# Sparse attention and two gated convolution layers: another order of a tile's transfers on the SyncE queue

## The chip, the core and the metric

The kernel runs on one core of one Trainium2 chip. The metric is the device time of one execution in microseconds. All work is issued by five engines that run side by side and meet only at semaphores: TensorE (PE), VectorE (DVE), ScalarE (ACT), GpSimd (POOL) and SyncE (SP), which here issues nearly all transfers between the chip's memory (HBM) and the on-chip memory.

## What is computed

`reference()` runs three layers one after the other. q, k and v have 2 batches, 8 heads, 768 rows and a head width of 64, in float32.

```
scores = scale * q @ k.T - slope[h] * dist              # keep: the first 8 keys and the last 96
a = exp(scores - max); a = a / (sum(a) + 1e-9); x = a @ v
x = (sigmoid(causal_conv5(x)) * (x @ w_val)) @ w_out    # layer 2, width 512
h = relu(x @ w_in)                                      # layer 3, width 1024
out = (h * sigmoid(conv3(h))) @ w_out2
```

The change touches only how the softmax's divisor, 1 / (sum(a) + 1e-9), travels to the result of attention, and when q, k and v are loaded.

## The kernel before

**Tiles.** Attention runs over TILES = 12 tiles of 128 query rows, tile t = 0 to 11, six for each batch. A tile has 8 heads (H) in 4 pairs (PAIRS). Its keys are 32 global ones, 96 of the previous tile and its own 128; tiles 0 and 6, the first of their batches, use their own 128 alone. q, k, v and the previous tile's rows of v stand in rings of RING = 4 slots, so tile t + 4 may be loaded when tile t has let go of its slot.

**The loop on each engine.** The order on every engine is written out by hand; no scheduler moves anything.

- PE, tile t: `qk(t + 1)` (scores of the next tile, L504), four `turn(t, j)` (transposes of the probabilities of tile t, L517), `pv(t)` (probabilities times v, L532). `pv(t)` takes the four pairs in turn and waits for each pair's copy of the turned probabilities, `probT`.
- DVE, tile t: `take_x(t - 1)` (L977, attention's result out of PSUM into `xT`), then the eight `score(t + 1, i)` (L954), and between them `inverse(t)` (L965 `total_eps`, L967 reciprocal), `turn_inverse(t)` (L973, a transpose of the inverses into `inv_rows`) and `copy_t1(t, 1)` (L961, the copy of pair 1 for which `pv(t)` waits). `copy_t1(t, 1)` stands behind `turn_inverse(t)`. Tiles 6 to 10 end with one or two steps of the first convolution (L982, `EARLY_STEPS`: 1, 2, 1, 2, 1), which read two operands from on-chip memory.
- ACT: eight exponentials of tile t + 1 (L701) and the copies of the other pairs (L708); from tile 5 on it copies pair 3 too.
- POOL, tile t: `key_window(t + 3)` (L389 and L390; waits for that tile's k), `split_w2` in tiles 0 to 3 or `split_x` in tiles 6 to 9 (L410, L412), then `scale_x(t - 1)` (L396, waits for the spread inverses `invT`; it multiplies them into `xT`, which is counted by `x_ready`).
- SP: the transfers, below.

**An inverse's way.** The inverses of a tile are 8 numbers for each of 128 query rows, one query row a partition. `xT` has the head's channels on the partitions, so they have to be turned and repeated. DVE transposes them into `inv_rows` (two slots, by t % 2). SP sends these rows to HBM, to `inv_turned` (L312, 16 KB; called the **send** below). When that has landed (semaphore `inv_sent`), SP reads them back twice, each time repeated over 64 partitions, into `invT` (L317, 2 x 128 KB; called the **spread**). DVE's `turn_inverse(t)` writes the slot that tile t - 2 sent from, and so waits until `inv_sent` of tile t - 2 has come.

**SP's queue.** It is in order: an instruction that waits holds up all behind it. For tile t it issues `load_q(t + 4)` (L293, waits for PE's `qk(t)`), `load_k(t + 4)` (L298, waits for the first half of `qk(t + 1)`), the send and the spread of tile t (`turn_inverse`), then `load_v(t + 4)` (L304, and for all but a batch's first tile L306 and L307; it waits for `pv(t)`). From tile 2 on the spread also waits for `scale_x(t - 2)`, the last reader of its slot.

**After attention** PE runs `val`, `hid` and `out` (products in three parts each, L561 to L563) to the end.

The functions that the change touches, with the lines of the profile:

Of the kernel before, what the change touches and what calls it, by code (L numbers as in the profile page):

```python
# [10 lines left out]
TILES = B * TPB  # L11
# [11 lines left out]
RING = 4  # L23
# [18 lines left out]
def program(nc, A_q, A_k, A_v, A_n, A_wval, A_w1t, A_win, A_w2, A_cw1, A_cw2, A_out):  # L42
# [7 lines left out]
    with ctx:  # L50
# [161 lines left out]
        def banded(eng):  # L212
            eng.wait_ge(n_in, 16)
            low_g, high_g, low_l, high_l = (eng.value_load(nw[0:1, i:i + 1]) for i in range(4))
            return (high_g == 0) & (high_l == 0) & (low_g >= 0) & (low_g <= GLOB) & (low_l >= 1) & (low_l <= PREV)
# [43 lines left out]
        def invT_of(t):  # L259
            return kW[:, 0, t % 2, :, :] if t >= LATE_INVERSES else invT[:, t % 2, :, :]  # L260

        def first_of_batch(t):
            return t % TPB == 0
# [16 lines left out]
        @block.sync  # L280
        def _(sp):
            sp.dma_start(win[:, 0, 0:F // 4], A_win[:, 0, 0:F // 4]).then_inc(start_in[0], 16)
            sp.dma_start(w1t[:, 0, P:C], A_w1t[:, 0, P:C]).then_inc(start_in[1], 16)
            for m in range(1, CT):
                sp.dma_start(w1t[:, m, :], A_w1t[:, m, :]).then_inc(w1_in[m], 16)
            sp.dma_start(wval, A_wval).then_inc(wv_in, 16)
            sp.dma_start(win[:, :, F // 2:F], A_win[:, :, F // 2:F]).then_inc(win_in, 16)


            def load_q(t):  # L290
                if t >= RING:
                    sp.wait_ge(qk_done, 2 * (t - RING) + 2)
                sp.dma_start(q_rows[:, t % RING, :, :], A_q[:, t, :, :]).then_inc(q_in[t % RING], 16)  # L293

            def load_k(t):
                if t >= RING:
                    sp.wait_ge(qk_done, 2 * (t - RING) + 3)
                sp.dma_start(kW[:, t % RING, 1, :, :], A_k[:, t, :, :]).then_inc(k_in[t % RING], 16)  # L298

            def load_v(t):  # L300
                if t >= RING:
                    sp.wait_ge(pv_done, t - RING + 1)
                slot = t % RING
                sp.dma_start(v_own[:, slot, :], A_v[:, t, :]).then_inc(v_in[slot], 16)  # L304
                if not first_of_batch(t):
                    sp.dma_start(v_win[GLOB:P, slot, :], A_v[GLOB:P, t - 1, :]).then_inc(v_in[slot], 16)  # L306
                    sp.dma_start(v_win[0:GLOB, slot, :], A_v[0:GLOB, t // TPB * TPB, :]).then_inc(v_in[slot], 16)  # L307

            def turn_inverse(t):
                slot = t % 2  # L310
                sp.wait_ge(inverse_done, t + 1)
                sp.dma_start(inv_turned[t].rearrange("h (b q) -> b h q", q=SQUARE), inv_rows[:, slot, :]).then_inc(inv_sent[slot], 16)  # L312
                sp.wait_ge(inv_sent[slot], 16 * (t // 2 + 1))
                if t >= 2:
                    sp.wait_ge(x_ready, t - 1)
                for e in range(2):
                    sp.dma_start(invT_of(t)[e * D:(e + 1) * D, :, :], inv_turned[t, e:H:2, :].partition_broadcast(D)).then_inc(invT_in[slot], 16)  # L317

            def load_w2(k):
                sp.dma_start(w2[:, k, :], A_w2[:, k, :]).then_inc(w2_in[k], 16)  # L320

            def general_load(m, first=False):
                tile = g_batch(m) * TPB
                pair = g_pair(m)
                if not first:
                    sp.wait_ge(g_pv, 2 * m)
                    sp.sem_inc(loading, 1)
                for e in range(2):
                    rows = slice(e * D, (e + 1) * D)
                    sp.dma_start(gq[:, e, :], A_q[rows, ds(tile + g_tile(m), 1), ds(pair, 1), :].rearrange("p t h s -> p (t h s)")).then_inc(g_in, 16)  # L330
                    sp.dma_start(gk[:, e, :, :], A_k[rows, ds(tile, TPB), ds(pair, 1), :].rearrange("p t h s -> p t (h s)")).then_inc(g_in, 16)
                sp.dma_start(gv[:, :, :], A_v[:, ds(tile, TPB), ds(2 * D * pair, 2 * D)]).then_inc(g_in, 16)

            with sp.If(banded(sp)):
                for t in range(RING):
                    load_q(t)
                    load_k(t)
                    load_v(t)
                for k in range(FT):
                    load_w2(k)  # L340
                for t in range(TILES):
                    if t + RING < TILES:
                        load_q(t + RING)
                        load_k(t + RING)
                    turn_inverse(t)
                    if t + RING < TILES:
                        load_v(t + RING)
            with sp.Else():
                sp.wait_ge(wvl_done, CT)
                general_load(0, first=True)  # L350
                for k in range(FT):
                    load_w2(k)
                with sp.Fori(1, G_STEPS) as m:
                    general_load(m)

            def store(c, ms):
                sp.wait_ge(o_free, CT * c + ms.stop)
                sp.dma_start(A_out[:, c, ms, :], ost(c)[:, ms, :]).then_inc(out_sent[c], 16)

            for c in range(CHUNKS - 1):  # L360
                store(c, slice(0, 2))
                store(c, slice(2, 4))
            store(CHUNKS - 1, slice(0, 2))
            store(CHUNKS - 1, slice(2, 3))
            store(CHUNKS - 1, slice(3, 4))
            for c in range(CHUNKS):
                sp.wait_ge(out_sent[c], 32 if c < CHUNKS - 1 else 48)
# [870 lines left out]
```

## Time and profile before

| | us |
|---|---|
| median of three runs | 277.49 |
| lowest, highest | 277.28, 278.51 |
| the profiled execution | 274.83 |
| its span, first to last instruction | 273.0 |
| PE busy | 261.7 (96%) |
| DVE busy | 185.8 (68%) |
| ACT busy | 155.3 (57%) |
| POOL busy | 47.7 (17%) |

All durations below come from the profiled execution, and times of day are microseconds from the start of its span. The busy shares are means over stages with different limits: attention ends at about 102 us, and the rest is PE's products. The rows on which the prediction rests are in a section of their own below.

### The profile page before, as it was taken

How to read it: one execution, taken by the hardware profiler on the slowest of the kernel's cores; microseconds unless marked ns; L12 is line 12 of the kernel's file. 1: busy time of each engine (PE TensorE's matmuls, PEld its weight loads, DVE VectorE, ACT ScalarE, POOL GpSimd, SP SyncE). 2: the span in 40 equal slices, each digit the busy share in tenths (PEclk: the TensorE clock that was granted, in tenths of full speed). 3: DMA queues.
4: the chain of work that ended last, by engine and by line, in shares of the span. 5: the costliest groups of instructions: out<-in, count | busy, mean ns of one | idle time of the engine just before them, and what ended most of it. 6: DMA issues, size and time to landing. Idle time of an engine off the chain costs nothing.

```text
span 273.0 us, 4415 instructions
## 1 busy us (share of the span) xinstructions
PE 261.7 (96%) x1526; PEld 205.4 (75%) x1526; DVE 185.8 (68%) x460; ACT 155.3 (57%) x353; POOL 47.7 (17%) x70
## 2 busy tenths in 40 slices
PE   8999999999977699999999999999999999999995
PEld 7444468888755588888888888888888888888883
DVE  0389399997966694698980696997508998992000
ACT  1051578889977686526451706765718748754110
POOL 1012095772254553400000000000000000000000
PEclk9999999999999999999999999999999999999999
DMA  6999716656554552100000000000000002104021
GB/s 196 365 379 316 289 42 197 194 162 182 160 158 133 169 145 83 45 0 0 2 0 0 0 2 0 0 0 1 2 0 0 0 2 87 67 0 155 1 90 64
DMA packets 20263, 25.16 MB, mean 92 GB/s; under 512 B 3728, under 2 KB 10384, under 8 KB 20112
## 3 DMA queue, kind: packets, MB, share of 16 engines
q1 hardware_dynamic: 19088, 23.86, 27.0%
q10 hardware_dynamic: 1152, 1.01, 1.1%
q8 instruction: 13, 0.21, 0.3%
q14 instruction: 10, 0.08, 0.1%
HBM read 21.52 MB, written 3.34 MB: 91 GB/s over the span
## 4 chain that ended last, share of the span: by engine, by line
PE 84%; DMA 8%; SPq 3%; DVE 2%; ACT 1%; issue 1%; ACTq 1%; DVEq 0%
PE ps L561 20%; PE ps L562 20%; PE ps L563 20%; PE ps L457 8%; PE ps L532 6%; PE ps L504 5%; PE ps L517 5%; DMA inv_turned<-inv_rows 4%; DMA win<-in_win 3%; SPq L317 1%; DVE prob L954 1%; SPq L304 0%; DVE probT L961 0%; SPq L298 0%; ACT prob L701 0%
## 5 line engine op out<-in xcount | busy, mean ns | idle before, releaser
L701 ACT ACTIVATE prob<-prob,low 128x256 f32<-128x256 f32 (+1 forms) x96 | 46.1, 483 | 10.5 <-DVE low L954 10.4
L982 DVE SCALAR_TENSOR_TENSOR g<-xT,cw,g 128x512 f32<-128x512 f32 x48 | 33.7, 767 | 1.6 <-ACT g L736 1.6
L810 ACT ACTIVATE h<-ps 128x512 f32<-128x512 f32 x24 | 14.0, 595 | 31.1 <-PE ps L563 31.1
L954 DVE CUSTOM_DVE_ANT_0 prob<-ps,bias 128x256 f32<-128x256 f32 x80 | 30.1, 409 | 1.7 <-PE ps L504 1.5
L561 PE MATMUL ps<-gh,Wh 128*128 128x512 f32 x64 | 24.9, 389 | 0.0
L562 PE MATMUL ps<-gl,Wh 128*128 128x512 f32 x64 | 24.9, 389 | 0.0
L563 PE MATMUL ps<-gh,Wl 128*128 128x512 f32 x64 | 24.9, 389 | 0.0
L561 PE MATMUL ps<-hghA,w2h 128*128 128x512 f32 x64 | 24.9, 389 | 0.0
L562 PE MATMUL ps<-hglA,w2h 128*128 128x512 f32 x64 | 24.9, 389 | 0.0
L563 PE MATMUL ps<-hghA,w2l 128*128 128x512 f32 x64 | 24.9, 389 | 0.0
L457 PE MATMUL ps<-win,w1t 128*128 128x512 f32 x56 | 24.7, 596 | 0.1
L1145 DVE SCALAR_TENSOR_TENSOR hgA<-h,cw,hgA 128x512 f32<-128x512 f32 x32 | 21.8, 745 | 3.6 <-ACT hgA L822 3.6
L517 PE MATMUL ps<-ident,prob 128*128 128x128 f32 x176 | 23.3, 278 | 0.6 <-ACT probT L708 0.5
L517 PEld LDWEIGHTS ps<-ident,prob 128*128 128x128 f32 x176 | 18.8, 140 | 5.9 <-issue 3.5
L504 PE MATMUL ps<-kW,q_rows 64*128 64x256 f32 (+1 forms) x192 | 22.3, 372 | 0.0
L532 PE MATMUL ps<-probT,v_win 128*64 128x128 f32 x160 | 16.3, 282 | 5.6 <-DVE probT L961 5.6
L457 PEld LDWEIGHTS ps<-win,w1t 128*128 128x128 f32 x56 | 10.5, 190 | 13.1 <-issue 12.0
L504 PEld LDWEIGHTS ps<-kW,q_rows 64*128 64x128 f32 x192 | 16.6, 186 | 4.6 <-issue 2.5
L708 ACT ACTIVATE probT<-ps 128x512 f32<-128x512 f32 (+1 forms) x31 | 17.2, 555 | 3.8 <-PE ps L517 3.7
L561 PE MATMUL ps<-xh,wvh 128*128 128x512 f32 x48 | 19.0, 396 | 0.0
L532 PE MATMUL ps<-probT,v_own 128*64 128x128 f32 x192 | 18.4, 276 | 0.6 <-DVE probT L961 0.4
L563 PE MATMUL ps<-xh,wvl 128*128 128x512 f32 x48 | 18.7, 390 | 0.0
(101 smaller groups left out, 530.6 us busy)
## 6 DMA issues: line engine op xcount, KB each, us to landing
q_rows<-in_q SPq DMA_DIRECT2D x12, 256.0 KB, 4.6
kW<-in_k SPq DMA_DIRECT2D x12, 256.0 KB, 4.4
v_own<-in_v SPq DMA_DIRECT2D x12, 256.0 KB, 3.7
invT<-inv_turned SPq DMA_DIRECT2D x20, 128.0 KB, 2.9
out<-xT SPq DMA_DIRECT2D x5, 512.0 KB, 2.8
w<-in_w SPq DMA_DIRECT2D x8, 256.0 KB, 10.0
v_win<-in_v SPq DMA_DIRECT2D x10, 192.0 KB, 3.4
prob<-in_wval SPq DMA_DIRECT2D x1, 1024.0 KB, 9.9
```

What stands on the lines that cost most here:

```text
L457: return pe.matmul(WB(i), w1t[:, m, k * P:(k + 1) * P], win[:, m, half * 512:(half + 1) * 512], start=(m == 0), stop=(m == CT - 1))
L504: last = pe.matmul(SC(f, i % 2)[:, i // 2, P if first_of_batch(t) else 0:KEYS], q_rows[rows, slot, pair, :], keys, start=True, stop=True)
L517: last = pe.transpose(PT(t, j)[:, (2 * i + c) * P:(2 * i + c + 1) * P], prob[:, t % 2, 2 * j + i, c * P:(c + 1) * P], ident[:, :])
L532: last = pe.matmul(PO[e * D:(e + 1) * D, j, :], v[:, slot, cols], probT[:, j // 2, j % 2 * 2 + e, c, :], start=(c == key_parts(t)[0]), sto ...
L561: pe.matmul(out, w_hi, x_hi, start=first, stop=False)
L562: pe.matmul(out, w_hi, x_lo, start=False, stop=False)
L563: return pe.matmul(out, w_lo, x_hi, start=False, stop=final)
L701: act.activation(part, part, ACT.Exp, scale=-1.0, bias=low[:, t % 2, i:i + 1], accum_out=total[:, t % 2, i:i + 1]).then_inc(exp_done, 1)
L708: act.activation(turned_to(t, j), turned(t, j), ACT.Copy).then_inc(t0_copied, 1)
L954: dve.tensor_tensor_reduce(prob[:, t % 2, i, cols], SC(f, e)[:, i % HH // 2, cols], table, -SCALE, 3.0e38, ALU.add, ALU.min, low[:, t % 2, ...
L982: dve.scalar_tensor_tensor(out=pieces(g[:, m, :], c), in0=x_cols(m, c, tap - PAD1), scalar=cw1[:, m, tap:tap + 1], in1=pieces(g[:, m, :], ...
L1145: dve.scalar_tensor_tensor(out=raw, in0=h_cols(m, c, tap - 1), scalar=cw2[:, m, tap:tap + 1], in1=raw, op0=ALU.mult, op1=ALU.add).then_inc ...
```

## The change

The transfers of a tile stand in another order on SP. Nothing is added or removed; the instructions on PE, DVE, ACT and POOL and their waits are as before.

```diff
-            def turn_inverse(t):
+            def send_inverse(t):
                 slot = t % 2
                 sp.wait_ge(inverse_done, t + 1)
                 sp.dma_start(inv_turned[t].rearrange("h (b q) -> b h q", q=SQUARE), inv_rows[:, slot, :]).then_inc(inv_sent[slot], 16)
+
+            def spread_inverse(t):
+                slot = t % 2
                 sp.wait_ge(inv_sent[slot], 16 * (t // 2 + 1))
                 if t >= 2:
                     sp.wait_ge(x_ready, t - 1)
...
                 for t in range(TILES):
+                    send_inverse(t)
+                    if t >= 1 and t - 1 + RING < TILES:
+                        load_v(t - 1 + RING)
                     if t + RING < TILES:
                         load_q(t + RING)
                         load_k(t + RING)
-                    turn_inverse(t)
-                    if t + RING < TILES:
-                        load_v(t + RING)
+                    spread_inverse(t)
```

The start of the loop on SP, tile 0 and tile 1, before:

```order
L293 DMA q_rows<-in_q 128x512 [waits qk_done]
L298 DMA kW<-in_k 128x512 [waits qk_done]
L312 DMA inv_turned<-inv_rows 4x32x32 [waits inverse_done]
L317 DMA invT<-inv_turned 64x4x128 [waits inv_sent0]
L317 DMA invT<-inv_turned 64x4x128
L304 DMA v_own<-in_v 128x512 [waits pv_done]
```

The same place after the change:

```order
L312 DMA inv_turned<-inv_rows 4x32x32 [waits inverse_done]
L293 DMA q_rows<-in_q 128x512 [waits qk_done]
L298 DMA kW<-in_k 128x512 [waits qk_done]
L320 DMA invT<-inv_turned 64x4x128 [waits inv_sent0]
L320 DMA invT<-inv_turned 64x4x128
L312 DMA inv_turned<-inv_rows 4x32x32 [waits inverse_done]
```

The send of tile 0 has moved ahead of the loads of q and k of tile 4, and the v of tile 4 now comes behind the send of tile 1.

From tile 1's spread to tile 2's, in the steady part of the loop on SP, before (the later tiles with loads have the same pattern; where the v is that of tile 6 it is L304 alone):

```order
L317 DMA invT<-inv_turned 64x4x128 [waits inv_sent1]
L317 DMA invT<-inv_turned 64x4x128
L304 DMA v_own<-in_v 128x512 [waits pv_done]
L306 DMA v_win<-in_v 96x512
L307 DMA v_win<-in_v 32x512
L293 DMA q_rows<-in_q 128x512 [waits qk_done]
L298 DMA kW<-in_k 128x512 [waits qk_done]
L312 DMA inv_turned<-inv_rows 4x32x32 [waits inverse_done]
L317 DMA invT<-inv_turned 64x4x128 [waits x_ready,inv_sent0]
L317 DMA invT<-inv_turned 64x4x128
```

The same place after the change:

```order
L320 DMA invT<-inv_turned 64x4x128 [waits inv_sent1]
L320 DMA invT<-inv_turned 64x4x128
L312 DMA inv_turned<-inv_rows 4x32x32 [waits inverse_done]
L304 DMA v_own<-in_v 128x512 [waits pv_done]
L306 DMA v_win<-in_v 96x512
L307 DMA v_win<-in_v 32x512
L293 DMA q_rows<-in_q 128x512 [waits qk_done]
L298 DMA kW<-in_k 128x512 [waits qk_done]
L320 DMA invT<-inv_turned 64x4x128 [waits x_ready,inv_sent0]
L320 DMA invT<-inv_turned 64x4x128
```

Before, nothing stood between a send and the spread that waits for its landing; now five loads do, and they wait for `inverse_done` of the tile in front of them.

## Rows read from the trace of the kernel before

**Rows 1.** The page, part 2: busy tenths of PE in 40 equal slices.

```profile
PE   8999999999977699999999999999999999999995
```

**Rows 2.** Stretches by engine: us, busy us (x instructions), PEclk, DMA share, GB/s.

```profile
72.00:96.00 24.00, 18.15 (x193) 14.54 (x192) 16.77 (x68) 18.74 (x63) 11.73 (x15) 1.00 0.56 168
...
112.00:270.00 158.00, 157.82 (x696) 130.32 (x695) 108.22 (x151) 79.36 (x110) 1.77 (x4) 1.00 0.05 20
```

**Rows 3.** Waits from 68 to 120 us: total us, times, longest.

```profile
DVE inv_rows L973 <- DMA inv_turned<-inv_rows: 6.9, 3, 2.3
...
PE ps L532 <- DVE probT L961: 5.6, 3, 2.1
```

**Rows 4.** Timeline of PE: start, us, instruction, idle time before it.

```profile
72.22 2.00 PE L504 MATMUL ps<-kW,q_rows 64*128 64x256 f32 x16
...
78.64 0.44 PE L532 MATMUL ps<-probT,v_win 128*64 128x128 f32 x4 [1.45 <-DVE probT L961]
...
96.32 2.00 PE L504 MATMUL ps<-kW,q_rows 64*128 64x256 f32 x16
...
102.30 0.50 PE L561 MATMUL ps<-xh,wvh 128*128 128x512 f32 x1
```

**Rows 5.** The chain of waits, 73 to 90 us: start, us, what.

```profile
73.49 3.88 DMA inv_turned<-inv_rows
...
77.38 0.61 SPq L317
...
78.03 0.62 SPq L317
...
78.70 0.60 SPq L304
...
79.34 0.43 SPq L306
...
79.81 0.43 SPq L307
...
80.29 0.42 SPq L293
...
80.75 0.43 SPq L298
...
81.23 4.17 DMA inv_turned<-inv_rows
```

**Rows 6.** Timeline of SP, the loads' part and the end of the loop.

```profile
73.01 0.43 SPq L298 DMA_DIRECT2D kW<-in_k  x1
...
100.31 0.55 SPq L312 DMA_DIRECT2D inv_turned<-inv_rows  x1
102.47 1.24 SPq L317 DMA_DIRECT2D invT<-inv_turned  x2
```

**Rows 7.** Timeline of DVE, tiles 7 to 10.

```profile
72.92 0.68 DVE L977 COPY xT<-ps 128x512 f32<-128x512 f32 x1
...
74.28 0.32 DVE L965 TENSOR_SCALAR total_eps<-total 128x8 f32<-128x8 f32 x1
...
77.46 0.21 DVE L973 STREAM_TRANSPOSE inv_rows<-inv 128x32 f32<-128x32 f32 x1 [2.33 <-DMA inv_turned<-inv_rows]
...
87.91 1.24 DVE L982 SCALAR_TENSOR_TENSOR g<-xT,cw,g 128x512 f32<-128x512 f32 x1
...
97.42 0.68 DVE L977 COPY xT<-ps 128x512 f32<-128x512 f32 x1
```

**Rows 8.** Timeline of POOL, the same tiles.

```profile
73.30 1.27 POOL L396 TENSOR_TENSOR xT<-xT,invT 128x512 f32<-128x512 f32 x1 [3.44 <-DMA invT<-inv_turned]
77.02 0.51 POOL L389 COPY kW<-kW 128x384 f32<-128x384 f32 x1 [2.45 <-DMA kW<-in_k]
...
80.99 1.44 POOL L396 TENSOR_TENSOR xT<-xT,invT 128x512 f32<-128x512 f32 x1 [1.31 <-DMA invT<-inv_turned]
...
87.32 1.27 POOL L412 TENSOR_TENSOR xl<-xT,xh 128x512 fp32r<-128x512 f32 x1
```

**Rows 9.** One line's instructions, L965 and L982 on DVE: ns min/median/max.

```profile
L965 DVE TENSOR_SCALAR total_eps<-total x12: 161/240/865, 36.2 to 104.0; 128x8 f32<-128x8 f32 x12
...
L982 DVE SCALAR_TENSOR_TENSOR g<-xT,cw,g x48: 736/750/1235, 72.3 to 164.9; 128x512 f32<-128x512 f32 x48
```

## The prediction

> **What bounds the kernel now.** I read the page first. PE is busy in nearly every tenth of every slice, except in three of the 40 slices, the 12th to the 14th, which read 7, 7, 6 [rows 1]. A slice is 6.8 us, so this is about 75 to 96 us, late in attention. The table of stretches says the same: from 72 to 96 us PE works 18.15 of 24.00 us, while from 112 to 270 us it works 157.82 of 158.00 at a granted clock of 1.00 [rows 2]. So behind attention nothing but PE's own work sets the time, and before it there is one hole of some 6 us. What closes the hole earlier makes the kernel shorter by as much, unless the later part loses its cover; that part moves as a whole (below).
>
> Who makes the hole? The waits say that `pv` on PE waited three times, 5.6 us in all, for DVE's copy of the turned probabilities (L961), and that DVE waited three times, 6.9 us, with `inv_rows` (L973) for the send to land [rows 3]. L973 stands in front of L961 on DVE, so these are the same three events: at 77.46 DVE comes out of 2.33 us of waiting, and at 78.64 PE comes out of 1.45 us [rows 7, 4]. The chain of waits then shows what the send waited for. It does not go back over PE at all between 73 and 94 us but runs round SP's queue: send 3.88, spread 0.61 and 0.62, v 0.60, 0.43, 0.43, q 0.42, k 0.43, and the next send at 81.23 [rows 5]. That is a closed ring of 81.23 - 73.49 = **7.74 us a tile** (the next one, with a landing of 4.17, is 8.01). PE needs less: its last tile of the loop, with no wait in it, takes 102.30 - 96.32 = **5.98 us** [rows 4]. SP is the slowest of the five in this loop. It falls behind by some 2 us with each tile; the two slots of `inv_rows` absorb that until tile 7, and from then on DVE and PE go at SP's pace for three tiles.
>
> **The change, part by part.** *The landing.* SP stood idle while a send landed. A send issued behind the loads took 3.88 and 4.17 us [rows 5]; with no load ahead of it 102.47 - 100.31 = 2.16 us [rows 6]. Now it goes in front, with only the last spread ahead, and I take 2.2 to 2.8, bounded by 4.2. Its cover is the issue of the five loads: 0.60 + 0.43 + 0.43 + 0.42 + 0.43 and gaps of 0.04, 2.5 us, and the send's own issue, 0.55 [rows 5, 6]. So SP reaches the spread 3.1 us after the send's start and waits for nothing or, at the upper bound, for 1.1 us. The spread costs 1.3. SP's period falls from 7.74 to **4.4 us (at most 5.5)**, under PE's 5.98 either way. SP now idles at `inverse_done`, and the send of tile t - 2 has landed some 9 us before DVE needs its slot. The three waits of DVE go.
>
> *What the five loads now wait behind.* They stand behind `inverse_done(t)`. On DVE `inverse(t)` follows `take_x(t - 1)`, which needs `pv(t - 1)`, and two scores of tile t + 1, which need the first half of `qk(t + 1)`. Those are the very events for which v, q and k wait, so no load waits for anything new except SP's turn. Tile 0 is the exception in time: q and k of tile 4, which could go at once, now follow the send of tile 0. `qk(4)` uses them three tiles later; at 4 us to land the price is nothing. In later tiles k is issued 2.65 us behind the send, and its window is copied some 4 us after its issue (73.01 to 77.02 [rows 6, 8]); `qk(t + 4)` comes over two tiles of PE behind send(t), at least 12 us, so 4 us or more of cover remain. v has more.
>
> *The spread, now behind the loads.* Before, it was used 80.99 - 77.38 = 3.6 us after its issue [rows 8, 5]. Behind a megabyte of loads I allow 3.6 to 5.5 us, the upper end by adding what loads ahead added to a send (4.0 - 2.2). It starts 3.1 us after the send instead of 3.9, so `invT` comes between 0.8 us earlier and 1.1 later in its tile. Its reader, `scale_x`, has nobody close behind: the next waiter for `x_ready` inside the loop is the spread two tiles on, about 11 us later, and the convolution's readers come later still. Zero on the path.
>
> *What is late next.* With SP gone, three tiles cost PE's 5.98 each instead of (96.32 - 72.22) = 24.10 us together [rows 4]: 24.10 - 17.94 = **6.16 us**. The idle records alone give 5.6 [rows 3], since a record begins where the modelled end of a matmul lies. But DVE is hardly faster than PE here. From 72.92 to 97.42 its three tiles take 24.50 us, less 6.9 of waits 17.6, or **5.87 us a tile** [rows 7, 3]. Only 0.1 us a tile is spare, and about 0.8 once, since 2.33 us of DVE's wait became 1.45 at PE.
>
> DVE's work is not of fixed length. A step of L982 takes 0.75 us at the median and 1.24 at 87.91, and that one ends just behind POOL's `xl` of 87.32 to 88.59. `total_eps` takes 0.16 at best, 0.87 at worst; that at 74.28 lasts 0.32 and ends just behind POOL's `scale_x` (73.30 to 74.57) [rows 7 to 9]. So these two kinds wait for a POOL instruction that runs. That costs 0.65 us in these tiles already, inside the 5.87. POOL's work in the stretch is 11.73 us for three tiles, 3.9 a tile [rows 2]: half of a tile of 8.0 us, but two thirds of one of 5.98. Where they now meet can be worked out roughly. k of tile t + 4 comes 6.7 us behind send(t); window, `xh` and `xl` are POOL's 3.9 without the 1.3 of `scale_x`, so `xl` (1.27 long) ends at 9.3 and `scale_x(t)` at 10.6. On DVE, L973 could have run at 77.46 - 2.33 = 75.13, so a send comes 1.1 us behind `total_eps` at 74.28; that of tile t + 2 thus stands 2 x 5.98 - 1.1 = 10.9 us behind send(t), `take_x` 1.4 earlier, at 9.5, and the convolution's steps just before it, from 8.1 (two steps) or 8.8. They hit `xl` almost squarely, and `total_eps` comes near the end of `scale_x`. I take half an instruction, 0.6 us, more in each of the tiles 7 to 9, 1.8 in all, less the 0.8 of once-spare time: **1.0 us** lost to PE, between 0 (they miss each other) and 3.5 (a meeting of 1.27 in full in each of three tiles, less 0.1 spare in each).
>
> The Trainium skill, "SBUF — State Buffer", section "SBUF: two separate sides", says that VectorE and GpSimd share a pair of ports as an exclusive lock: a VectorE instruction with two operands in on-chip memory, or in a two-port mode, and a GpSimd instruction shut each other out for a whole instruction. The trace agrees where rows were shown. If every meeting counted in full, as the rule would have it when phases lock, the sum would be that of the slow rival below; by the durations in the trace alone, which already hold 0.65 us of it, the sum would be a gain of 6.1.
>
> *Behind attention* nothing is edited. DVE, ACT and PE enter it in the same relation as before. The last tiles have no loads, so there SP's order is the old one, and with less of a lag carried into it the inverses arrive earlier relative to PE, not later. Zero.
>
> **Sum.** 6.1 - 1.0 = 5.1 us. The profiled execution goes from 274.83 to 269.7 (its span of 273.0 has 1.8 us around it, which stays). It lies 2.66 below the median; the same subtraction from 277.49 gives **272.4 us**.
>
> **The rivals.**
>
> *Clean recovery.* DVE and POOL miss each other, or the spare time absorbs what they lose. For it: three tiles of before hold only 0.65 us of such delays, and 0.8 is spare. Against: POOL's denser tile. Gain 6.1, time 271.4.
>
> *The queue stays the limit.* The send is slow not because loads stand ahead of it but because its own pattern (16 KB in 128-byte runs) shares the transfer engines with whatever runs, now the loads behind it. For it: the DMA share is 0.56 and will be about 0.75 in the shorter tiles. Against: at a landing of 4.2 SP's period is still 5.5, below PE's. It takes 4.7 us to equal 5.98, and about 6.7 to leave no gain, which no send in the trace took. At 6.3 us the period is 7.6 and the gain 3 x (24.10 / 3 - 7.6) = 1.3: 276.2.
>
> *Slower: DVE becomes the bound through POOL.* In tiles 7 to 10 there are four `total_eps` and four groups of L982. If each meets a POOL instruction at its start, they lose 8 x 1.27 = 10.2 us; less 0.8 spare this outweighs the 6.1, and the kernel is slower by 3.3: 280.8. It decides at a sum of 6.9 us of such waits, against 0.65 now. Since POOL follows DVE round the same loop, the phases could lock, but POOL is free a third of the time.
>
> *Slower by late loads* would need k to land over 10 us after its issue, against 4.0.
>
> **How the numbers follow.** The forecast (0.5 to 3.5 us lost, 271.8 to 274.9) has 0.58, clean recovery 0.31, the queue as the limit 0.07, slower 0.02, and 0.02 is left for what I don't see (such as a granted clock below 1.00 once PE has no hole, which nothing in 112 to 270 us supports). The range must take in clean recovery with half a microsecond of the runs' spread, 270.9, and the upper end of the loss, 274.9. A measurement can tell about 0.5%, 1.4 us, from no change: faster by more has 0.93, within it 0.05, slower 0.02.
>
> **What the next profile shows.** The page's slices 12 to 14 of PE read 9. The wait of L973 for `inv_turned` is gone from DVE's list, and SP's long waits are for DVE's `inv_rows` instead of its own send. The send's landing, read as the start of the spread, is no more than about 3.1 us after the send. DVE's tiles 7 to 9 last 6.0 to 6.5 us, with single L982 or L965 stretched; if the sum of that stretching is near zero, the loss of 1.0 was wrong. PE's first L561 starts at about 97.2 instead of 102.30. If it starts there and the time is nonetheless unchanged, then the part behind attention was not PE's alone. A spread still waiting 3 us or more for its send would show the queue rival right.

## The result and the profile after

| us | before | after |
|---|---|---|
| median of the first comparison (4 executions each) | 277.38 | 269.58 |
| lowest, highest | 276.95, 278.51 | 268.26, 271.33 |
| median over the experiments' 95 executions of the kernel before, and all 10 of the changed one | 276.36 | 269.58 |
| the profiled execution | 274.83 | 269.20 |
| its span | 273.0 | 267.3 |

The ratio of the first comparison is 0.9717, with a 95% interval of 0.9652 to 0.9781. The direction was right, but 269.58 lies 1.3 us below the range that was given (270.9 to 274.9), so the prediction of 272.4 was wrong. The profiled executions differ by 5.63 us, close to the 5.1 that were worked out (0.3 of the 5.63 is an earlier start of attention, `qk(0)` at 25.49 instead of 25.81, which is there before SP's order differs); the medians differ by 6.7 to 7.8. Finding that difference is what most of the experiments were for. Below, medians of one job (executions timed together on one chip) are compared with each other, slower and faster executions alike, since the kernel before scatters over some 5 us. Of its 96 executions in the experiments one, more than twice as long as the others, is left out.

What answers to [rows 1] is the busy tenths of PE in 40 slices, after the change:

```profile
PE   8999999999999999999999999999999999999995
```

The hole is gone. What answers to [rows 2] (a stretch, its us, then busy us of PE, PEld, DVE, ACT and POOL, the granted clock, the share and rate of the transfers) shows PE at work for 23.66 of 24 us instead of 18.15, and POOL's work packed into the same stretch, 16.65 us instead of 11.73:

```profile
72.00:96.00 24.00, 23.66 (x254) 19.23 (x252) 23.67 (x95) 22.59 (x79) 16.65 (x19) 1.00 0.57 160
```

SP's own waits (engine and line, what it waited for, us in total, times, longest), first one row of before, then two after the change:

```profile
SPq L317 <- DMA inv_turned<-inv_rows: 30.5, 12, 3.5
...
SPq L312 <- DVE inv_rows L977: 29.9, 10, 14.4
SPq L320 <- DMA inv_turned<-inv_rows: 7.0, 6, 1.4
```

Before, SP waited 30.5 us, twelve times, for its own sends to land. Now that is 7.0 us, and SP waits for DVE instead (14.4 of the 29.9 us ahead of tile 0's send): it is no longer the slowest. DVE's wait for its slot [rows 3] is not in its list any more. One piece of SP's timeline, tile 7's (start, us, transfers), and the start of tile 8's:

```profile
75.59 0.55 SPq L312 DMA_DIRECT2D inv_turned<-inv_rows  x1
76.19 0.46 SPq L304 DMA_DIRECT2D v_own<-in_v  x1
76.69 0.43 SPq L306 DMA_DIRECT2D v_win<-in_v  x1
77.16 0.43 SPq L307 DMA_DIRECT2D v_win<-in_v  x1
77.63 0.42 SPq L293 DMA_DIRECT2D q_rows<-in_q  x1
78.10 0.43 SPq L298 DMA_DIRECT2D kW<-in_k  x1
80.03 1.25 SPq L320 DMA_DIRECT2D invT<-inv_turned  x2
82.39 0.56 SPq L312 DMA_DIRECT2D inv_turned<-inv_rows  x1
```

The five loads stand in the time in which the send lands. The landing itself is not short here: 80.03 - 75.59 = 4.44 us. This send follows at once on a spread that itself stands behind loads. Tile 5's, which does too, took 4.2 us, while tile 8's, issued 1.1 us after the spread in front of it, took at most 2.6. But 2.9 of the 4.4 are now covered, and SP is free at 81.3, a microsecond before DVE has the next inverses.

PE's timeline (start, us, line, tile) answers to [rows 4]:

```profile
72.50 2.00 PE L508 MATMUL ps<-kW,q_rows 64*128 64x256 f32 x16
...
90.80 2.00 PE L508 MATMUL ps<-kW,q_rows 64*128 64x256 f32 x16
96.69 0.50 PE L565 MATMUL ps<-xh,wvh 128*128 128x512 f32 x1
```

The three tiles that took 24.10 us take 90.80 - 72.50 = 18.30. The products start at 96.69 instead of 102.30 and run for 170.6 us to the end, as before (170.7).

### The profile page after: what moved, and what is told of

It is laid out like the page before. It is cut to its first block, busy times and chain, and to the rows that moved or that the text cites. A ratio compares the mean times of both kernels' runs of the same rounds, so it can differ in the third digit from the quotient of the medians.

```text
span 267.3 us, 4415 instructions
## 1 busy us (share of the span) xinstructions
PE 261.8 (98%) x1526; PEld 205.5 (77%) x1526; DVE 187.4 (70%) x460; ACT 154.8 (58%) x353; POOL 47.9 (18%) x70
## 4 chain that ended last, share of the span: by engine, by line
PE 89%; DMA 3%; DVE 2%; ACT 2%; issue 1%; ACTq 1%
PE ps L565 21%; PE ps L566 20%; PE ps L567 20%; PE ps L461 8%; PE ps L536 8%; PE ps L521 6%; PE ps L508 6%; DMA win<-in_win 3%; ACT prob L705 1%; DVE prob L958 1%; DVE total_eps L969 1%; ACT probT L712 0%; DVE probT L965 0%; ACT Wh L693 0%; ACT xT L837 0%
## 5 line engine op out<-in xcount | busy, mean ns | idle before, releaser
L566 PE MATMUL ps<-xl,wvh 128*128 128x512 f32 x48 | 18.7, 390 | 0.0
```

Of the source, the lines that this page charges most:

```text
L566: pe.matmul(out, w_hi, x_lo, start=False, stop=False)
```

## The experiments

**The kernel before, once more** (`b_again`, no edit).

> The kernel before, unchanged, to learn why its timed runs (median 277.4 us) lie 2.6 us above its profiled execution (274.83 us), while the changed kernel's do not (269.58 against 269.20). Theory A: the kernel before goes round SP's queue from tile 1 on, so a longer landing of each send is added some seven times over; in executions at 277 us the sends land 0.3 to 0.4 us later than in the profiled one (4.3 to 4.5 us instead of 3.9 to 4.2) and the whole difference lies before PE's first L561 (102.3 us then, about 105 now). Rival B: the offset belongs to the launch or the chip and is spread over the whole kernel; then the part behind attention, 170.7 us from the first L561 to the end of the span, is longer too.

Measured: 276.39 us (12 executions), beside 276.48 for 23 others of the same job. Its profiled execution took 275.32, and there the products start at 102.81 and last 170.7 us, so rival B is out: the part behind attention is not longer. But theory A was not right either. From tile 1's send to tile 7's it is 45.5 us, no more than the 45.9 of the profile shown ahead of the prediction. What is new is the granted clock, in the stretches from 90 us on (us, busy of the five, clock, transfers):

```profile
90.00:92.00 2.00, 1.81 (x19) 1.28 (x17) 0.16 (x2) 2.00 (x7) 0.00 (x0) 1.00 0.59 200
92.00:94.00 2.00, 0.00 (x0) 0.00 (x0) 1.29 (x5) 1.00 (x3) 1.86 (x4) 0.93 0.05 14
94.00:96.00 2.00, 1.99 (x20) 1.99 (x22) 2.00 (x10) 1.67 (x7) 0.71 (x1) 0.50 0.77 164
96.00:98.00 2.00, 2.00 (x18) 1.57 (x18) 1.35 (x2) 0.40 (x2) 1.90 (x2) 0.72 0.66 229
98.00:100.00 2.00, 2.00 (x20) 1.62 (x17) 1.85 (x7) 1.05 (x3) 1.62 (x2) 1.00 0.16 46
```

PE has no matmul from 92 to 94 us, in tile 9's hole; behind it the clock is 0.50, that is 1.2 instead of 2.4 GHz, and it is back by 98 us. Half speed shows in the matmuls too (PE's timeline, idle time in brackets):

```profile
91.42 0.39 PE L532 MATMUL ps<-probT,v_own 128*64 128x128 f32 x4
94.01 0.70 PE L532 MATMUL ps<-probT,v_win 128*64 128x128 f32 x4 [2.20 <-DVE probT L961]
94.49 0.64 PE L532 MATMUL ps<-probT,v_own 128*64 128x128 f32 x4
```

The profiled execution that the prediction was made from had a hole of the same length and no fall (PE's timeline of it, and below it where the products start in `b_again`):

```profile
94.86 0.44 PE L532 MATMUL ps<-probT,v_win 128*64 128x128 f32 x4 [2.15 <-DVE probT L961]
...
102.81 0.50 PE L561 MATMUL ps<-xh,wvh 128*128 128x512 f32 x1
```

From the end of tile 9's hole to the products the same matmuls take 102.30 - 94.86 = 7.44 us without the fall [rows 4] and 102.81 - 94.01 = 8.80 with it: behind this last hole the fall costs **1.4 us**. The execution without a fall was the exception. Each execution's mean granted clock is known; over the 95 executions of the kernel before in this study:

| mean granted clock | executions | median us |
|---|---|---|
| 0.998 and more | 14 | 274.25 |
| 0.991 to 0.994 (one fall, as in `b_again`'s profile at 0.994) | 63 | 276.25 |
| under 0.991 (two, as in `b_late`'s profile at 0.986) | 18 | 277.62 |

Of the ten executions of the changed kernel none is under 0.999.

**One more transfer a tile** on SP, in the kernel before (`b_late`; the tile `spare` and the semaphore are new too).

```diff
                     turn_inverse(t)
+                    sp.dma_start(spare[:, 4 * t:4 * t + 4], A_cw1[:, 0, 0:4]).then_inc(spare_in, 16)
```

> The kernel before with one more small transfer issued on SP in each tile, behind the spread (some 0.45 us of issue). It computes the same. Theory A (the ring of SP's queue is closed from tile 1 on, though PE waits only in tiles 7 to 9): six rings and more carry the extra issue, +2.7 to +3.3 us. Rival: only the three tiles in which PE waits pay for it, +1.4 us.

Measured: 280.38 against 276.48, +3.9 us. The issue took 0.60 us instead of the 0.45 assumed; with its gap that is 0.64, and six rings carry 3.8. The rival's three tiles would have paid 1.9. All four executions of this kernel have a mean clock under 0.991, that is more falls than most of the kernel before, so the time alone would leave some doubt. The sends do not: from tile 1's to tile 7's it is 49.3 us (44.01 to 93.28) instead of 45.9. So the ring is closed from tile 1 on, long before PE waits.

This profile also shows what a fall costs that has another hole behind it. The clock falls to 0.50 behind the hole of 3.14 us in tile 7 and again behind that of 2.39 in tile 9, but between them (PE's timeline, and DVE's in the middle row):

```profile
82.37 0.44 PE L535 MATMUL ps<-probT,v_win 128*64 128x128 f32 x4 [3.14 <-DVE probT L964]
...
89.05 0.21 DVE L976 STREAM_TRANSPOSE inv_rows<-inv 128x32 f32<-128x32 f32 x1 [1.02 <-DMA inv_turned<-inv_rows]
...
90.23 0.44 PE L535 MATMUL ps<-probT,v_win 128*64 128x128 f32 x4 [0.20 <-DVE probT L964]
```

In tile 8 PE is idle for only 0.20 us, since the slow stretch has filled the time in which it would have waited. But DVE still waits 1.02 us for a send to land, so SP sets the pace of this tile, fall or no fall. There the fall costs nothing that the trace shows.

**The same transfer in the changed kernel** (`a_late`, between the send and v).

> The changed kernel with the same additional small transfer a tile on SP that cost the kernel before 3.9 us (b_late, 280.38 against 276.48), here between send and v. It computes the same. If SP is off the path, the 0.6 us more of issue disappear in its idle time: 269.2 to 270.0. If SP still sets the pace: +3 us or more.

Measured: 270.09 us, 0.5 above the changed kernel's 269.58: a seventh of what it costs in the kernel before, and hardly above the scatter. SP is off the path.

**Four slots instead of two** (`b_slots4`, SP's order as before).

```diff
-        inv_rows = sb("inv_rows", [P, 2, SQUARE], where=am)
+        inv_rows = sb("inv_rows", [P, 4, SQUARE], where=am)
...
-                if t >= 2:
-                    dve.wait_ge(inv_sent[t % 2], 16 * (t // 2))
+                if t >= 4:
+                    dve.wait_ge(inv_sent[t % 4], 16 * (t // 4))
...
```

> The kernel before with four slots of inv_rows instead of two, so that DVE waits for the send of four tiles back; the order on SP is that of before. Theory A (the queue's period of some 8 us is the bound, and DVE's wait only the place where it shows): DVE's wait goes, but k for tiles 10 and 11 is now issued too late, POOL's key window and then qk wait for it, and the time stays within 1.5 us of before. Rival C (the wait of DVE for its slot is the cause): the time falls by the same 5.6 to 7.8 us as with the change.

Measured: 274.78 us, 1.7 below its job's 276.48, a little more than expected, and about a quarter of the change's gain. (SP's send and the wait for it use the four slots too.) In its profile it is 45.7 us from tile 1's send to tile 7's, so the ring is that of before. The products start at 102.31; that is where they did in the profile of before, which had no fall, while this one has one (clock 0.50 at 96 to 98 us). DVE no longer waits for its slot, and PE waits in another place (PE's timeline, all its waits for POOL):

```profile
86.21 2.00 PE L505 MATMUL ps<-kW,q_rows 64*128 64x256 f32 x16 [1.63 <-POOL kW L391]
94.81 3.68 PE L505 MATMUL ps<-kW,q_rows 64*128 64x256 f32 x16 [2.71 <-POOL kW L391]
```

Tiles 10 and 11 lack their keys, because the late queue issued k too late. The wait that the profile of before names was not the cause; it was the first of several by which the queue's 8 us a tile can reach PE.

**The spread directly behind its send** (`s_spread_first`: send, spread, v, q, k).

```diff
                     send_inverse(t)
+                    spread_inverse(t)
...
-                    spread_inverse(t)
```

> The changed kernel with the spread put back directly behind its send, so the order is send, spread, v, q, k. Theory A (what helps is that the loads are issued while the send lands): the ring is that of before turned by a few places, some 7.7 us, and the time is that of before within 1.5 us. Rival D (what helps is that the send goes ahead of the tile's loads): the send lands in 2.2 to 2.8 us, the ring is 6.2 us, and most of the gain, 4 us or more, stays.

Measured: 279.66 us, 3.2 above before. Rival D is out: a send in front of its own tile's loads, but with nothing between it and its spread, still stands behind the last tile's loads, and its landing is not covered. Two of its sends in SP's timeline:

```profile
72.57 0.57 SPq L312 DMA_DIRECT2D inv_turned<-inv_rows  x1
76.54 1.26 SPq L320 DMA_DIRECT2D invT<-inv_turned  x2
...
80.39 0.57 SPq L312 DMA_DIRECT2D inv_turned<-inv_rows  x1
84.05 1.26 SPq L320 DMA_DIRECT2D invT<-inv_turned  x2
```

The ring is 7.8 us with a landing of 4.0. I had not expected it to be slower than before. Its waits point at k, which is issued later relative to its tile than before: PE waits for POOL's key window five times, 8.7 us, from tile 6 on.

**Half of the change** (`s_cover_v`: q, k, send, v, spread).

```diff
-                    send_inverse(t)
-                    if t >= 1 and t - 1 + RING < TILES:
-                        load_v(t - 1 + RING)
                     if t + RING < TILES:
                         load_q(t + RING)
                         load_k(t + RING)
+                    send_inverse(t)
+                    if t >= 1 and t - 1 + RING < TILES:
+                        load_v(t - 1 + RING)
                     spread_inverse(t)
```

> Half of the change: q and k stay ahead of the send as before, only v stands between send and spread. The send still lands in about 4 us behind two loads. Ring: 4.0 + 1.3 + 0.9 = 6.2 to 6.3 us against PE's 5.8 to 6.0. If it is only the ring's period against PE's that counts, the lag grows by 0.3 us a tile and never reaches DVE's slot: the whole gain, 268.5 to 270.5. If the send's early place is what matters, most of the hole stays: 273 or more.

Measured: 268.61 us (268.06 to 269.93) against 269.57 for the full change in its job, all of the gain; 1.0 us between two so small groups is within their scatter. SP still waits 12.3 us for its sends in this kernel, and it does not matter. Half of the loads as cover suffice to bring the ring down to PE's period.

**The hole filled, in the kernel before** (`b_fill`, and `b_fill2` with less). PE repeats the products of pair 0 before it waits for pair 1.

```diff
+FILL = {7: 3, 8: 4, 9: 4}
...
-                for j in range(PAIRS):
+                for j in [0] * FILL.get(t, 0) + list(range(PAIRS)):
```

> The kernel before, with TensorE kept at work in its hole: in tiles 7, 8 and 9 pv computes pair 0 three or four times over (1.3 to 1.8 us) before it waits for pair 1's copy. The numbers that come out are the same. Theory E (the hole itself costs more than its length: after 1.6 to 2.3 us without work the granted clock falls to 1.2 GHz for some 3.3 us, as at 94 us in the repeated kernel before, and this happens in most executions but did not in the profiled one of before): mean clock 1.000 in nearly all runs, median 274.5 to 275.0 against 276.5, so 1.5 to 2 us faster though SP's ring is untouched. Rival F (the falls of the clock have nothing to do with the hole): clock 0.994 and 276.4 as before, or slower by the added work.

> As b_fill, with less added work: pair 0 computed again 2, 2 and 3 times in tiles 7, 8 and 9 (0.9, 0.9 and 1.3 us), so that in most executions all of it lies inside PE's wait and the rest of the wait is about 1 us. Theory E: a wait of 1 us does not bring the clock down; mean clock 0.998 to 1.000, and since the added work is free this time, the median is 1.2 to 1.8 us under the kernel before of the same job. Rival G: the fall costs little because SP's ring, not PE, sets the pace where it falls; then the clock is 1.000 and the time within 0.6 us of before.

Measured: 275.85 against 276.26, and 275.87 against 276.24. The clock was 0.998 or more in 21 of the 24 executions, against 14 of 95 without filling: an idle PE is what brings the clock down. But only 0.4 us came back in each, not the 1.2 to 2 expected, and rival G's two signs, the clock at 1.000 in most executions and the time within 0.6 us of before, are what `b_fill2` shows. `b_late`'s first fall shows where G holds: while SP's ring sets the pace. It does not hold behind the last hole (`b_again`, 1.4 us). The 0.4 cannot decide how much of that came back: the interval of `b_fill2`'s ratio, 0.9948 to 1.0029, reaches from 1.4 us gained to 0.8 lost. Nor do the 2.0 us between the first two rows of the table of clocks give the price of a fall, since executions with long holes are slow because of the hole, and have the falls too.

**One hole made on purpose** in the changed kernel (`a_hole`; the semaphore `again` is new), and the same hole filled (`a_hole_fill`, with `FILL = {9: 5}` as above).

```diff
+                for n in range(4 if t == 9 else 0):
+                    dve.tensor_copy(turned_to(t, j), turned(t, j)).then_inc(again, 1)
+                    dve.wait_ge(again, n + 1)
                 dve.tensor_copy(turned_to(t, j), turned(t, j)).then_inc(t1_copied, 1)
```

> The changed kernel with a hole made on purpose: in tile 9 DVE makes its copy for pair 1 five times instead of once (the same numbers), some 2.6 to 3 us more, so that PE stands idle for about 2.2 us at one place, as in tile 9 of the kernel before, but with no ring of SP's that scatters. Theory E: the clock falls behind it, mean 0.994, and the time is that of the next kernel plus the price of the fall. Rival F: clock 1.000.

> The same hole on DVE, filled on PE: pair 0 of tile 9 is computed again five times (2.2 us) ahead of the wait. Same numbers. Both kernels are late by the same copies, so what is between them is the fall of the clock alone: 1.2 to 1.6 us if the column of mean clocks of the kernel before tells the price (274.6 us at 1.00, 276.25 at 0.994), 0.3 to 0.6 if the filled kernels before (275.8) do.

Measured: 273.79 and 273.50 us; the clock was under 0.995 in 6 of 11 executions with the hole and in none of 11 with the filled one. From PE's timeline, first the hole:

```profile
93.42 0.69 PE L537 MATMUL ps<-probT,v_win 128*64 128x128 f32 x4 [2.82 <-DVE probT L969]
...
102.11 0.50 PE L566 MATMUL ps<-xh,wvh 128*128 128x512 f32 x1
```

and the filled one:

```profile
93.21 0.44 PE L538 MATMUL ps<-probT,v_win 128*64 128x128 f32 x4 [0.80 <-DVE probT L970]
...
100.93 0.50 PE L567 MATMUL ps<-xh,wvh 128*128 128x512 f32 x1
```

The same work takes 8.69 us behind the hole and 7.72 behind the filled one: a fall costs **1.0 us** here. (It would be more than that, near the 1.4 of `b_again`, if the filled kernel did not wait once more for DVE in tile 10, 0.20 us at 99.47, a wait that the slow stretch hides in the other.) Within `a_hole`, the executions with a fall have a median of 274.4 and the five without 273.1, 1.3 us apart. The medians of the two kernels differ by only 0.3, less than these say, since half of the executions had no fall and each scatters by 1 us; among other things attention starts at 27.7 us in the profile of the one and at 26.0 in that of the other.

**The changed kernel, once more** (`a_again`).

> The changed kernel, unchanged, in more executions. Theory E: no hole, so the clock is 1.000 in nearly all, and the median is 268.5 to 270, 7 us or so under before's 276.5, of which 5.6 are the stalls and the rest the clock. Rival: the 7.8 us between the two medians was scatter of four runs, and the difference is the 5.6 of the profiled executions.

Measured: 269.57 us against 276.26 in its job, 6.7 us. The gain is more than the 5.6 of the profiled executions, and less than the 7.8 of the first comparison, some of which was scatter.

**Without `total_eps`**, in the changed kernel (`a_noeps`), in the kernel before (`b_noeps`), and in the half change (`c_noeps`).

```diff
-                dve.tensor_scalar(total_eps[:, :], total[:, t % 2, :], 1e-9, None, ALU.add).then_inc(total_done, 1)
-                dve.wait_ge(total_done, t + 1)
-                dve.reciprocal(inv[:, 0:H], total_eps[:, :]).then_inc(reciprocal_done, 1)
+                dve.reciprocal(inv[:, 0:H], total[:, t % 2, :]).then_inc(reciprocal_done, 1)
```

> The changed kernel without total_eps: the reciprocal is taken of the total itself, and the 1e-9 is left out (it is under half a unit in the last place of a total of 1 or more, so the numbers are the same). This takes away from DVE the instruction that waited 1.12 and 1.04 us for POOL in tiles 8 and 9 of the changed kernel. If those waits reach PE, tiles 7 to 9 go from 6.2, 6.1, 6.0 us towards 5.8, and the time falls by 0.3 to 0.9 us. If spare time absorbs them, no change.

> The kernel before without total_eps (the edit that made the changed kernel 1.7 us faster, 269.57 to 267.87). The 1e-9 is left out of the divisor. If SP's ring is the bound, DVE's time saved in each tile is lost again in its wait for the slot, and only what tile 0 gains (its send goes 0.6 us earlier, total_eps took 0.56 there) is kept: 0.4 to 0.8 us under before. If VectorE's delays counted in both kernels, it would gain 1.7 here too.

> s_cover_v (q and k ahead of the send, v between send and spread) without total_eps. s_cover_v had 268.61 against 269.57 of the full change, and total_eps was worth 1.7. If the two add up: 266.9 to 267.4. If both took away the same thing, VectorE's waits for POOL in tiles 3 to 9, it is a_noeps again: 267.6 to 268.2.

Measured: 267.87 against 269.57 (-1.7), 275.73 against 276.24 (-0.5, which is within the scatter), and 268.21. The profiles say where it comes from. From `qk(1)` to `qk(2)` it is 5.17 us in the kernel before and in the changed one, and 4.57 in both without `total_eps`: 0.6 us either way. From there to the products the changed kernel goes from 57.9 to 56.8 us, 1.1 less. The kernel before shows no gain there (64.2 in `b_noeps`, 64.2 in `b_again`, each with one fall), and its DVE still waits four times, 1.7 to 2.1 us each, for a send. So beside these 0.6 us at tile 0's inverses the edit is worth 1.1 us where SP's ring is gone and, by these profiles, nothing where it stands. The 1.7 is more than the 0.3 to 0.9 that I had expected of tiles 7 to 9 alone, by tile 0 and by what `total_eps` loses in earlier tiles (changed kernel, ns, min/median/max):

```profile
L969 DVE TENSOR_SCALAR total_eps<-total x12: 159/542/1183, 35.8 to 98.5; 128x8 f32<-128x8 f32 x12
```

Its median was 240 ns before [rows 9] and is 542 now: it waits for POOL in tiles 2 to 4 as well. `a_noeps` is the fastest version of the study, 267.87 us; `c_noeps` is no better than it, which fits that the two edits take away the same waits; with six executions each it is not shown.

## Why the prediction was right and wrong

- *What bounds the kernel* was right: the queue's period and not DVE's slot. `b_late`, `b_slots4` and `s_spread_first` each show it in another way, and `a_late` shows that it is over.
- *The landing* was mis-sized. I took 2.2 to 2.8 us and at most 4.2; it is 2.0 for tile 0 but 4.4 for tile 7, where in quick succession the send stands behind a spread that stands behind loads. The round of the queue that it allows is 4.44 + 1.3 = 5.7 us, above the stated bound of 5.5. The step held nonetheless, but by 0.2 us: 5.7 is still under PE's 5.98. The spread's 3.6 to 5.5 us, the loads' cover and the zero for the part behind attention all held (k takes about 5 us to its window instead of 4).
- *What is late next* was right in kind and too high in size. It gave 1.0 us for tiles 7 to 9; they lost 0.36 (they fell by 5.80 of the clean 6.16 us). The tiles ahead of them, which I had left out, lost 0.6 (from `qk(2)` to the `qk` at 72.50 it is 33.68 us, before 33.09), with `total_eps` longer in tiles 2 to 4. That the two make up the 1.0 us of the forecast is luck. One row shows such a meeting (DVE's timeline):

```profile
80.58 1.12 DVE L969 TENSOR_SCALAR total_eps<-total 128x8 f32<-128x8 f32 x1
```

It ends at 81.70, and POOL's `xl` (L416, 80.39 to 81.67) has just ended. The Trainium skill, "SBUF — State Buffer", section "SBUF: two separate sides", has it that of two such instructions the one that comes second fully blocks while the other holds the pair; this row agrees. The convolution's steps, which I had expected to be hit as well, were hit hardly at all (0.75 us each, one pair 1.46 instead of 1.41); once it was POOL that lasted longer, `xl` at 84.61 with 1.83 us instead of 1.28, begun just behind the step at 84.57.

- *The step that failed* is the last of the sum, "the same subtraction from 277.49 gives 272.4". It took the 2.66 us between the profiled execution and the median for something constant that lies around the kernel. It does not. 1.1 us of it was chance: the three executions with the median 277.49 lay above the 276.4 of the 95 later ones. The rest belonged, in part at least, to the hole that the change removes. In five of six executions of the kernel before, PE's clock falls to 1.2 GHz behind a hole once or twice, and the profiled one had escaped that. A fall costs 1.4 us behind the last hole (`b_again`), 1.0 in `a_hole`, and nothing visible where SP still sets the pace of the next tile (`b_late`). The changed kernel has neither hole nor falls, and its median lies 0.4 us above its profiled execution. Applied to 274.83, the same sum gave 269.7; 269.20 was measured, 0.3 of the difference being the earlier start of attention.
- I had given 0.02 to "a granted clock below 1.00 once PE has no hole". The clock did matter, but the other way round: it fell because of the hole.

What stays open: of the 1.6 us by which the median of before (276.4) exceeds the profiled 274.83, one fall behind the last hole explains 1.0 to 1.4, but in how many executions the fall comes there is not known. The rest may be longer holes or later starts of attention (its first L504 at 25.3 to 27.8 us in the profiles); the profiles are too few to share it out. Filling the holes brought back 0.4 us, less than a fall and within the scatter; in those kernels the added work lies in the path whenever a hole is shorter than it, and how much that took was not measured.

## What to carry to other kernels

A queue that waits in order for its own transfer to land should issue whatever is ready between the issue and the wait; count the queue's period per tile against the slowest engine's, because slots only postpone the stall, and removing the wait that the profile names only moves it. Where a stall is long, ask what it does to the clock behind it, and whether another wait follows that absorbs the slow stretch, and do not carry the distance between a profiled execution and the median over to the changed kernel: a part of it may belong to what is removed. Once a queue stops being the bound, small delays between two engines that cost nothing before (`total_eps` beyond tile 0) come to count (1.1 us).

## What the runs showed of the hardware

- A pause of PE of some 1.5 to 3 us was followed by a stretch at 1.2 GHz in most executions but not in all (none behind the 1.45, 1.96 and 2.15 us of the profile of before): 6 of 11 with one made hole, 81 of 95 with three natural ones, 3 of 24 when they were filled. Where it came it lasted about 3.4 us (an estimate from 0.93, 0.50 and 0.72 over three stretches of 2 us) and cost 1.0 to 1.4 us, or nothing visible where the next tile waited for SP anyway.
- A send of 16 KB took 2.0 to 2.2 us to land with no load shortly ahead of it, 3.3 to 4.2 behind a tile's loads in the kernel before, and 4.4 behind a spread and loads in the changed one.
- A VectorE instruction of 0.16 us took up to 1.18 us beside GpSimd's, and a GpSimd one of 1.28 us took 1.83 beside VectorE's.
